# A retention stage with its output one chunk behind its state and scores, ahead of a mixture of experts

## The chip, the cores and the metric

The kernel runs on one core of one Trainium2 chip. The metric is the time of one execution on the device in microseconds (us). The time before is the median of three runs, 659.53 us (658.33 to 659.57).

## The reference

q, k and v are (2 batches, 8 heads, 576 positions, 64). Retention is attention with a decay in place of the softmax; a mixture of 4 experts and one more layer with a Mish-like activation follow.

```python
gamma = 1 - 2 ** (-5 - arange(H))                      # one decay per head
D = where(i >= j, gamma ** (i - j), 0)                 # i, j positions
x = matmul((q @ k.T) / 8 * D, v)                       # -> (1152 tokens, 512)
p = domain_probs / (domain_probs.sum(-1) + 1e-9)
x = sum(p[:, e] * (relu(x @ w1[e]) @ w2[e]) for e in range(4))   # 512 -> 1024 -> 512
h = x @ w_in                                           # 512 -> 2048
out = (h * tanh(softplus(h))) @ w_out                  # 2048 -> 512
```

## The kernel before

**The stages.** The program has two stages. The retention stage goes through 18 chunks of 64 tokens (9 for each batch). The matrix stage works through 144 tiles of 128 hidden features by 384 tokens, each with 12 matmuls into a hidden bank and then 12 that project it (`project`, `project_tokens`). Each product of two fp32 numbers is made of three matmuls of rounded parts (`three`, lines 314 to 316): hi by hi, hi by lo, lo by hi. For each weight tile ("half") ACT makes the part w_hi (`unit_hi`, L212) and POOL then w_lo (`unit_lo`, L218); for the tokens ACT makes x_hi (L442) and VectorE x_lo (L494).

**One chunk.** `qkv` has 8 slots. The first 64 partitions (KEYS) of a slot hold v and k by position; the other 64 (FEATS) hold k and q by feature. TensorE multiplies k and q for the scores (`scores_head`, L268), into one of two banks. POOL multiplies v by its decay (`v_decay`, L636), for which it needs the chunk and the constants. VectorE masks the scores and writes them over k in the slot (`masked`, L479), once the state's matmuls have read k. The state is the running sum of k times v, one matmul per head (`state_head`, L272), accumulated in bank 2 over a batch. ACT copies it into the next slot over k by feature (`state_copy`, L409), once the next chunk's scores have read that. So a slot then holds state over v and q over masked scores, and the output is one matmul per head with 128 rows (`output`, L308). VectorE scales it to `x_tmp` (`decayed`, L488), ACT and VectorE split it in x_hi and x_lo (`first_lo`). `row_decay` (L591) makes a table that the scaling uses, one row ahead.

**The order.** Each engine's queue is written out by hand and runs in order, with semaphores between them. TensorE's turn c (L386 to L391) is: scores of chunk c+1 with the state of chunk c, head by head in alternation (`scores_and_state`); output of chunk c. From turn 7 on, halves of hidden tiles of the matrix stage (`hidden_half`, 6 matmuls each) stand in it, after the scores (AFTER_SCORES) and after the output (AFTER_OUTPUT): two a turn in turns 7 to 11, one in turns 12 to 17. VectorE's turn c is masked(c), a row of row_decay, first_lo(c-1), the hidden tiles' work (`lo`, `moe_act`), decayed(c). ACT's turn c is state_copy(c), x_hi(c-1), in turn 2 a wait for the probabilities' write and a DMA, then the w_hi that SPLIT_IN gives this turn and the h_hi. POOL's turn c is v_decay(c+1) and then the w_lo of SPLIT_IN, weight tiles 0 to 7 in turns 6 to 12. The SP queue loads chunk 0, the constants (214 KB), chunks 1 to 6, weight tiles 0 and 1, and then chunks and weight tiles in turn; from chunk 8 on each chunk waits for the output of the chunk 8 before it.

**Its end.** After turn 17 TensorE does a whole hidden tile (`hidden_products(8)`), and the first `project` waits for a drain of VectorE (L604) behind decayed(17), first_lo(17) and moe_act(7).

Of the kernel before, what the change touches and what calls it, by code (L numbers as in the profile page):

```python
# [13 lines left out]
P = 128  # L14
# [28 lines left out]

ROW0 = PAIRS * CH
STEP0 = ROW0 + PER_BATCH * PAIRS
KEY0 = STEP0 + PER_BATCH * HEADS
CONSTS = KEY0 + CH

# [5 lines left out]
def states(c):  # L54
# [3 lines left out]

AFTER_SCORES = {7: (0, 0), 8: (1, 0), 9: (2, 0), 10: (3, 0), 11: (4, 0),
                12: (5, 0), 13: (5, 1), 14: (6, 0), 15: (6, 1), 16: (7, 0), 17: (7, 1)}
AFTER_OUTPUT = {7: (0, 1), 8: (1, 1), 9: (2, 1), 10: (3, 1), 11: (4, 1)}
HIDDEN_IN = {t: c for turns in (AFTER_SCORES, AFTER_OUTPUT) for c, (t, half) in turns.items() if half}

SPLIT_IN = {0: 6, 1: 6, 2: 7, 3: 8, 4: 9, 5: 10, 6: 11, 7: 12, 8: 16, 9: 17, 10: 18}

# [14 lines left out]
def build(nc, chunks_in, consts_in, probs_in, weights_in, probs_dram, out):  # L82
    with ExitStack() as ctx:
# [41 lines left out]

        row0 = consts[:, 0:ROW0].rearrange("p (h c) -> p h c", h=PAIRS)
        row_step = consts[:, ROW0:STEP0].rearrange("p (c h) -> p c h", h=PAIRS)
        key_decay = consts[:, STEP0:KEY0].rearrange("p (c h) -> p c h", h=HEADS)
        mask = consts[KEYS, KEY0:CONSTS]

        banks = [ctx.enter_context(nc.psum_tensor(f"bank{i}", [P, 512], F32)) for i in range(8)]
        ps_s = [banks[i][KEYS, :].rearrange("p (h c) -> p h c", h=HEADS) for i in range(2)]
        ps_state = banks[2][FEATS, :].rearrange("p (h c) -> p h c", h=HEADS)
        ps_o = banks[3][:, 0:PAIRS * CH].rearrange("p (h c) -> p h c", h=PAIRS)
# [4 lines left out]
        s_slot = [sem(f"s_slot{i}") for i in range(SLOTS)]  # L139
        s_const = sem("s_const")  # L140
        s_zt = sem("s_zt")
        s_vd = sem("s_vd")
# [81 lines left out]
        def _(sp):  # L224
# [10 lines left out]
            load_chunk(0)  # L235
            sp.dma_start(consts[:, :], consts_in).then_inc(s_const, 16)
            for c in range(1, 7):
                load_chunk(c)
            load_half(0)
            for u in range(1, UNITS):  # L240
                load_half(u)
                load_chunk(6 + u)
# [23 lines left out]
        def _(pe):  # L266
            def scores_head(c, h):
                return pe.matmul(ps_s[c % 2][:, h], by_feats(c, 0)[:, h], by_feats(c, 1)[:, h],  # L268
                                 start=True, stop=True)

            def state_head(c, h):
                return pe.matmul(ps_state[:, h], by_keys(c, 1)[:, h], by_keys(c, 0)[:, h],  # L272
                                 start=(c % PER_BATCH == 0 and h == 0), stop=True, skip_group_check=True)

            def scores_and_state(c):

                n = c + 1
                if n < CHUNKS:
                    pe.wait_ge(s_slot[n % SLOTS], landed(n))
                    if n >= 2:  # L280
                        pe.wait_ge(s_sm, n - 1)
                if has_state(c):
                    pe.wait_ge(s_vd, c + 1)
                    if c > 0:
                        pe.wait_ge(s_st, states(c - 1))
                for h in range(HEADS):
                    if n < CHUNKS:
                        mm = scores_head(n, h)
                        if h == HEADS - 1:
                            mm.then_inc(s_sc, 1)  # L290
                    if has_state(c):
                        mm = state_head(c, h)
                        if h == HEADS - 1:
                            mm.then_inc(s_kv, 1)

            def output(c):

                pe.wait_ge(s_vd, c + 1)
                pe.wait_ge(s_sm, c + 1)
                rows = KEYS  # L300
                if c % PER_BATCH > 0:
                    rows = slice(0, P)
                    pe.wait_ge(s_st, states(c - 1))
                if c > 0:
                    pe.wait_ge(s_xt, c)
                for hp in range(PAIRS):
                    for x in range(2):
                        mm = pe.matmul(ps_o[DH * x:DH * (x + 1), hp], qkv[rows, c % SLOTS, 0, 2 * hp + x],  # L308
                                       qkv[rows, c % SLOTS, 1, 2 * hp + x], start=True, stop=True)
                mm.then_inc(s_o, 1)  # L310
# [73 lines left out]
            mm.then_inc(s_sc, 1)  # L384
            for c in range(CHUNKS):
                scores_and_state(c)  # L386
                if c in AFTER_SCORES:
                    hidden_half(*AFTER_SCORES[c])
                output(c)
                if c in AFTER_OUTPUT:  # L390
                    hidden_half(*AFTER_OUTPUT[c])  # L391
# [10 lines left out]
        def _(act):  # L402
# [3 lines left out]
            def state_copy(c):  # L406
                act.wait_ge(s_sc, c + 2)
                act.wait_ge(s_kv, states(c))
                act.activation(by_feats(c + 1, 0), ps_state, ACT.Copy).then_inc(s_st, 1)  # L409

# [25 lines left out]

            for c in range(CHUNKS + 1):
                if c < CHUNKS and has_state(c):
                    state_copy(c)
                if c > 0:  # L440
                    act.wait_ge(s_xt, c)
# [31 lines left out]
        def _(dve):  # L473
            def masked(c):

                dve.wait_ge(s_sc, c + 1)
                if has_state(c):
                    dve.wait_ge(s_kv, states(c))
                dve.tensor_tensor(by_keys(c, 1), ps_s[c % 2], mask.unsqueeze(1).broadcast_to([CH, HEADS, CH]),  # L479
                                  ALU.mult).then_inc(s_sm, 1)  # L480
# [105 lines left out]

            for c in range(CHUNKS + 1):
                if c < CHUNKS:
                    masked(c)
                if c < PER_BATCH - 1:  # L590
                    dve.tensor_tensor(row_decay[:, c + 1], row0,  # L591
                                      row_step[:, c + 1].unsqueeze(2).broadcast_to([P, PAIRS, CH]), ALU.mult)\
                       .then_inc(s_rd, 1)
                if c > 0:
                    first_lo(c - 1)
                for t, turn in HIDDEN_IN.items():
                    if turn + 2 == c:
                        lo(t)
                for t, turn in HIDDEN_IN.items():
                    if turn + 1 == c:  # L600
                        moe_act(t)
                if c < CHUNKS:
                    decayed(c)
            dve.drain().then_inc(s_af, KT)  # L604
# [55 lines left out]
def tables():  # L660
# [3 lines left out]
    c = np.arange(PER_BATCH, dtype=np.float64)  # L664
    consts = np.zeros((P, CONSTS))
    rows = gamma[:, None] ** (i[None, :] - MID) / np.sqrt(DH)
    consts[:, 0:ROW0] = np.repeat(rows.reshape(PAIRS, 2, CH).transpose(1, 0, 2), DH, axis=0).reshape(P, ROW0)
    steps = gamma[:, None] ** (CH * c[None, :])
    steps = np.repeat(steps.reshape(PAIRS, 2, PER_BATCH).transpose(1, 2, 0), DH, axis=0)
    consts[:, ROW0:STEP0] = steps.reshape(P, STEP0 - ROW0)  # L670
    keys = gamma[None, None, :] ** (MID - CH * c[None, :, None] - i[:, None, None])
    consts[KEYS, STEP0:KEY0] = keys.reshape(CH, KEY0 - STEP0)
    consts[KEYS, KEY0:CONSTS] = i[:, None] <= i[None, :]
    return consts.astype(np.float32)
# [32 lines left out]
```

## Time and profile before

| | |
|---|---|
| median of three runs | 659.53 us (658.33 to 659.57) |
| profiled execution | 655.74 us, of it 653.9 us span |
| TensorE (PE) busy | 638.8 us, 98% |
| VectorE (DVE) busy | 357.3 us, 55% |
| ScalarE (ACT), GpSimd (POOL) | 219.7 us, 204.4 us |
| granted TensorE clock | 0.999 of full speed |
| retention stage | to about 65.4 us |

PE is TensorE's matmuls, PEld its weight loads, which overlap them. Times in the trace count from the start of the span. A matmul's end is modelled and matmuls overlap, so of a run of them the starts are what to read. A fp32 matmul leaves two records: 8 matmuls show as x16. In a row "[2.90 <-DMA x]" is idle time of the engine ahead of the instruction and what ended it.

### The profile page before, as it was taken

What the parts mean: (1) busy time and instruction counts of PE and PEld (TensorE: products, weight loads), DVE (VectorE), ACT (ScalarE), POOL (GpSimd) and SP (SyncE); (2) the same over time, 40 slices, a digit from 0 to 9 for tenths busy, and PEclk for the clock granted to TensorE, in tenths of its full rate; (3) what the DMA queues carried; (4) which work ended last, traced back from release to release, by engine and by line L of the source; (5) the groups of instructions that cost most, each with busy time, mean ns of one, the idle gap of its engine ahead of it and who ended that gap; (6) DMA issues with size and microseconds to landing.
All of it is one profiled execution on the core that took longest, in us unless ns stands there. A gap on an engine that the chain in (4) does not pass through costs nothing.

```text
span 653.9 us, 10358 instructions
## 1 busy us (share of the span) xinstructions
PE 638.8 (98%) x4153; PEld 609.8 (93%) x4153; DVE 357.3 (55%) x624; ACT 219.7 (34%) x431; POOL 204.4 (31%) x167
## 2 busy tenths in 40 slices
PE   6799999999999999999999999999999999999998
PEld 4688999999999999999999999999998999999986
DVE  4757333232423232424242324348999999999772
ACT  2445312222212212212212212336554655565540
POOL 5464402222212212211212211224443555553220
PEclk9999999999999999999999999999999999999999
DMA  8854311111111201111111110111110111001001
GB/s 335 337 187 143 97 33 49 49 34 49 49 33 33 65 33 48 50 33 34 48 49 49 50 32 25 57 33 34 48 49 17 49 48 34 2 1 48 1 33 65
DMA packets 19232, 40.25 MB, mean 62 GB/s; under 512 B 2672, under 2 KB 2928, under 8 KB 19184
## 3 DMA queue, kind: packets, MB, share of 16 engines
q1 hardware_dynamic: 18368, 39.35, 19.1%
q8 instruction: 33, 0.54, 0.3%
q10 hardware_dynamic: 816, 0.23, 0.2%
q14 instruction: 15, 0.12, 0.1%
HBM read 37.20 MB, written 2.38 MB: 61 GB/s over the span
## 4 chain that ended last, share of the span: by engine, by line
PE 85%; DVE 9%; DMA 2%; issue 2%; ACT 1%; POOL 0%; SPq 0%; ACTq 0%; DVEq 0%
PE bank L314 28%; PE bank L316 27%; PE bank L315 27%; DVE m_n L568 2%; PE bank L268 2%; DVE m_a L556 1%; DVE m_w L558 1%; DMA probs_by_expert<-p_norm 1%; PE bank L308 1%; DVE m_c L565 1%; DVE h_lo L500 1%; DMA qkv<-in_chunks 1%; DVE x_lo L547 1%; DVE acc_sb L542 0%; ACT qkv L409 0%
## 5 line engine op out<-in xcount | busy, mean ns | idle before, releaser
L218 POOL TENSOR_TENSOR w_lo<-w_raw,w_hi 128x512 fp32r<-128x512 f32 x96 | 129.5, 1350 | 305.1 <-ACT w_hi L212 305.1
L314 PE MATMUL bank<-x_hi,w_hi 128*128 128x384 f32 x576 | 194.7, 338 | 0.5 <-POOL w_lo L218 0.5
L316 PE MATMUL bank<-x_hi,w_lo 128*128 128x384 f32 x576 | 193.0, 335 | 0.0
L315 PE MATMUL bank<-x_lo,w_hi 128*128 128x384 f32 x576 | 192.7, 335 | 0.0
L416 ACT ACTIVATE h_hi<-h_act 128x384 fp32r<-128x384 f32 x144 | 75.6, 525 | 305.7 <-PE bank L316 266.6
L500 DVE TENSOR_TENSOR h_lo<-h_act,h_hi 128x384 fp32r<-128x384 f32 x144 | 83.4, 579 | 164.5 <-ACT h_hi L416 163.8
L314 PE MATMUL bank<-h_hi,w_hi 128*128 128x384 f32 x384 | 128.3, 334 | 0.0
L315 PE MATMUL bank<-h_lo,w_hi 128*128 128x384 f32 x384 | 128.3, 334 | 0.0
L316 PE MATMUL bank<-h_hi,w_lo 128*128 128x384 f32 x384 | 128.3, 334 | 0.0
L314 PEld LDWEIGHTS bank<-x_hi,w_hi 128*128 128x128 f32 x576 | 108.1, 188 | 3.4 <-issue 0.6
L315 PEld LDWEIGHTS bank<-x_lo,w_hi 128*128 128x128 f32 x576 | 108.1, 188 | 1.7
L316 PEld LDWEIGHTS bank<-x_hi,w_lo 128*128 128x128 f32 x576 | 108.1, 188 | 0.0
L513 DVE SCALAR_TENSOR_TENSOR h_act<-bank,pb 128x384 f32<-128x384 f32 x96 | 53.4, 557 | 78.2 <-PE bank L316 78.2
L642 POOL TENSOR_TENSOR m_t<-m_w,m_r 128x384 f32<-128x384 f32 x48 | 55.6, 1159 | 117.3 <-ACT m_r L435 117.3
L314 PEld LDWEIGHTS bank<-h_hi,w_hi 128*128 128x128 f32 x384 | 72.1, 188 | 0.2 <-issue 0.2
L315 PEld LDWEIGHTS bank<-h_lo,w_hi 128*128 128x128 f32 x384 | 72.1, 188 | 0.0
L316 PEld LDWEIGHTS bank<-h_hi,w_lo 128*128 128x128 f32 x384 | 72.1, 188 | 0.0
L212 ACT ACTIVATE w_hi<-w_raw 128x512 fp32r<-128x512 f32 x96 | 59.1, 618 | 17.8 <-PE bank L316 17.8
L314 PE MATMUL bank<-w_hi,h_hi 128*128 128x512 f32 x144 | 56.2, 390 | 1.3 <-DVE acc_sb L540 1.1
L316 PE MATMUL bank<-w_hi,h_lo 128*128 128x512 f32 x144 | 56.8, 395 | 0.0
L315 PE MATMUL bank<-w_lo,h_hi 128*128 128x512 f32 x144 | 56.7, 394 | 0.0
L558 DVE SCALAR_TENSOR_TENSOR m_w<-m_u,m_a 128x384 f32<-128x384 f32 x48 | 42.4, 882 | 1.7
(42 smaller groups left out, 492.8 us busy)
## 6 DMA issues: line engine op xcount, KB each, us to landing
w_raw<-in_weights SPq DMA_DIRECT2D x96, 256.0 KB, 2.7
qkv<-in_chunks SPq DMA_DIRECT2D x18, 512.0 KB, 6.6
pb<-probs_by_expert SPq DMA_DIRECT2D x3, 576.0 KB, 6.0
out<-acc_sb SPq DMA_DIRECT2D x2, 768.0 KB, 4.5
out<-acc_sb SPq DMA_DIRECT2D x3, 256.0 KB, 2.1
pb<-probs_by_expert SPq DMA_DIRECT2D x1, 384.0 KB, 5.3
consts<-in_consts SPq DMA_DIRECT2D x1, 214.0 KB, 3.8
pb<-probs_by_expert ACTq DMA_DIRECT2D x1, 192.0 KB, 7.1
```

What stands on the lines that cost most here:

```text
L212: act.activation(w_hi[:, part, u], w_raw[:, half % RAW], ACT.Copy).then_inc(s_wh, 1)
L218: pool.tensor_tensor(w_lo[:, part, u], w_raw[:, half % RAW], w_hi[:, part, u].bitcast(F32), ALU.subtract).then_inc(s_wl, 1)
L268: return pe.matmul(ps_s[c % 2][:, h], by_feats(c, 0)[:, h], by_feats(c, 1)[:, h], start=True, stop=True)
L314: pe.matmul(out, w[0], x[0], start=first, stop=False)
L315: pe.matmul(out, w[0], x[1], start=False, stop=False)
L316: return pe.matmul(out, w[1], x[0], start=False, stop=last)
L416: act.activation(h_hi[:, n % UNITS, :], h_act[:, n % 2, :], ACT.Copy).then_inc(s_hh, 1)
L500: dve.tensor_tensor(h_lo[:, n % UNITS, :], h_act[:, n % 2, :], h_hi[:, n % UNITS, :].bitcast(F32), ALU.subtract).then_inc(s_hl, 1)
L513: dve.scalar_tensor_tensor(h_act[:, n % 2, :], ps_h[n % HR], 0.0, pb[:, e, cols(c)], ALU.max, ALU.mult).then_inc(s_hf, 1)
L558: dve.scalar_tensor_tensor(m_w[:, n % 2, :], m_u[:, n % 2, :], MISH_CAP, m_a[:, :], ALU.min, ALU.mult).then_inc(s_w, 1)
L568: dve.scalar_tensor_tensor(m_n[:, :], m_c[:, :], 2.0, m_t[:, n % 2, :], ALU.subtract, ALU.mult).then_inc(s_mn, 1)
L642: pool.tensor_tensor(m_t[:, n % 2, :], m_w[:, n % 2, :], m_r[:, n % 2, :], ALU.mult).then_inc(s_t, 1)
```

## The change

TensorE's turn c issues the output of chunk c-1 rather than c, so there are 19 turns. The hidden halves, ACT's and VectorE's turns follow by one. Scores have three banks (0 to 2) rather than two. The state lies in banks 0 and 1 (four heads each, on the partitions that the scores don't use) rather than bank 2, ACT copies it in two instructions, and TensorE waits for the first ahead of head 0 and for the second ahead of head 4. VectorE does decayed(c-1) right behind masked(c), and row_decay and first_lo after it. The constants load in two DMAs: key decay and mask (64 partitions, 35 KB) ahead of chunk 1, the rest behind it. Weight tile 0 is loaded ahead of chunk 6, and split in turn 5. Of the diff, the function that lays out the constants' table on the host is left out.

```diff
--- before.py
+++ after.py
@@ -41,10 +41,11 @@
 MISH_CAP = float(np.exp(20.0))
 
 
-ROW0 = PAIRS * CH
-STEP0 = ROW0 + PER_BATCH * PAIRS
-KEY0 = STEP0 + PER_BATCH * HEADS
-CONSTS = KEY0 + CH
+
+MASK0 = PER_BATCH * HEADS
+ROW0 = MASK0 + CH
+STEP0 = ROW0 + PAIRS * CH
+CONSTS = STEP0 + PER_BATCH * PAIRS
 
 
 def has_state(c):
@@ -57,13 +58,18 @@
 
 
 
-
-AFTER_SCORES = {7: (0, 0), 8: (1, 0), 9: (2, 0), 10: (3, 0), 11: (4, 0),
-                12: (5, 0), 13: (5, 1), 14: (6, 0), 15: (6, 1), 16: (7, 0), 17: (7, 1)}
-AFTER_OUTPUT = {7: (0, 1), 8: (1, 1), 9: (2, 1), 10: (3, 1), 11: (4, 1)}
+TURNS = CHUNKS + 1
+SCORES = 3
+HS = HEADS // 2
+
+
+
+AFTER_SCORES = {8: (0, 1), 9: (1, 1), 10: (2, 1), 11: (3, 1), 12: (4, 1), 13: (5, 0), 14: (5, 1),
+                15: (6, 0), 16: (6, 1), 17: (7, 0), 18: (7, 1)}
+AFTER_OUTPUT = {7: (0, 0), 8: (1, 0), 9: (2, 0), 10: (3, 0), 11: (4, 0)}
 HIDDEN_IN = {t: c for turns in (AFTER_SCORES, AFTER_OUTPUT) for c, (t, half) in turns.items() if half}
 
-SPLIT_IN = {0: 6, 1: 6, 2: 7, 3: 8, 4: 9, 5: 10, 6: 11, 7: 12, 8: 16, 9: 17, 10: 18}
+SPLIT_IN = {0: 5, 1: 6, 2: 7, 3: 8, 4: 9, 5: 10, 6: 11, 7: 12, 8: 16, 9: 17, 10: 18}
 
 
 def split_steps():
@@ -123,14 +129,14 @@
         m_c = sb("m_c", [P, TC])
         m_n = sb("m_n", [P, TC])
 
-        row0 = consts[:, 0:ROW0].rearrange("p (h c) -> p h c", h=PAIRS)
-        row_step = consts[:, ROW0:STEP0].rearrange("p (c h) -> p c h", h=PAIRS)
-        key_decay = consts[:, STEP0:KEY0].rearrange("p (c h) -> p c h", h=HEADS)
-        mask = consts[KEYS, KEY0:CONSTS]
+        key_decay = consts[:, 0:MASK0].rearrange("p (c h) -> p c h", h=HEADS)
+        mask = consts[KEYS, MASK0:ROW0]
+        row0 = consts[:, ROW0:STEP0].rearrange("p (h c) -> p h c", h=PAIRS)
+        row_step = consts[:, STEP0:CONSTS].rearrange("p (c h) -> p c h", h=PAIRS)
 
         banks = [ctx.enter_context(nc.psum_tensor(f"bank{i}", [P, 512], F32)) for i in range(8)]
-        ps_s = [banks[i][KEYS, :].rearrange("p (h c) -> p h c", h=HEADS) for i in range(2)]
-        ps_state = banks[2][FEATS, :].rearrange("p (h c) -> p h c", h=HEADS)
+        ps_s = [banks[i][KEYS, :].rearrange("p (h c) -> p h c", h=HEADS) for i in range(SCORES)]
+        ps_state = [banks[i][FEATS, 0:HS * DH].rearrange("p (h c) -> p h c", h=HS) for i in range(2)]
         ps_o = banks[3][:, 0:PAIRS * CH].rearrange("p (h c) -> p h c", h=PAIRS)
         ps_acc = [banks[d][:, 0:TC] for d in range(KT)]
         ps_out = [banks[tt][:, :] for tt in range(TT)]
@@ -138,6 +144,7 @@
 
         s_slot = [sem(f"s_slot{i}") for i in range(SLOTS)]
         s_const = sem("s_const")
+        s_rows = sem("s_rows")
         s_zt = sem("s_zt")
         s_vd = sem("s_vd")
         s_sc = sem("s_sc")
@@ -233,11 +240,12 @@
                 sp.dma_start(w_raw[:, half % RAW], weights_in[half]).then_inc(s_raw[half % RAW], 16)
 
             load_chunk(0)
-            sp.dma_start(consts[:, :], consts_in).then_inc(s_const, 16)
-            for c in range(1, 7):
+            sp.dma_start(consts[KEYS, 0:ROW0], consts_in[KEYS, 0:ROW0]).then_inc(s_const, 16)
+            load_chunk(1)
+            sp.dma_start(consts[:, ROW0:], consts_in[:, ROW0:]).then_inc(s_rows, 16)
+            for c in range(2, 6):
                 load_chunk(c)
-            load_half(0)
-            for u in range(1, UNITS):
+            for u in range(UNITS):
                 load_half(u)
                 load_chunk(6 + u)
             for c in range(6 + UNITS, CHUNKS):
@@ -265,25 +273,25 @@
         @block.tensor
         def _(pe):
             def scores_head(c, h):
-                return pe.matmul(ps_s[c % 2][:, h], by_feats(c, 0)[:, h], by_feats(c, 1)[:, h],
+                return pe.matmul(ps_s[c % SCORES][:, h], by_feats(c, 0)[:, h], by_feats(c, 1)[:, h],
                                  start=True, stop=True)
 
             def state_head(c, h):
-                return pe.matmul(ps_state[:, h], by_keys(c, 1)[:, h], by_keys(c, 0)[:, h],
-                                 start=(c % PER_BATCH == 0 and h == 0), stop=True, skip_group_check=True)
+                return pe.matmul(ps_state[h // HS][:, h % HS], by_keys(c, 1)[:, h], by_keys(c, 0)[:, h],
+                                 start=(c % PER_BATCH == 0 and h % HS == 0), stop=True, skip_group_check=True)
 
             def scores_and_state(c):
 
                 n = c + 1
                 if n < CHUNKS:
                     pe.wait_ge(s_slot[n % SLOTS], landed(n))
-                    if n >= 2:
-                        pe.wait_ge(s_sm, n - 1)
+                    if n >= SCORES:
+                        pe.wait_ge(s_sm, n - SCORES + 1)
                 if has_state(c):
                     pe.wait_ge(s_vd, c + 1)
-                    if c > 0:
-                        pe.wait_ge(s_st, states(c - 1))
                 for h in range(HEADS):
+                    if has_state(c) and c > 0 and h % HS == 0:
+                        pe.wait_ge(s_st, 2 * states(c - 1) - 1 + h // HS)
                     if n < CHUNKS:
                         mm = scores_head(n, h)
                         if h == HEADS - 1:
@@ -300,7 +308,7 @@
                 rows = KEYS
                 if c % PER_BATCH > 0:
                     rows = slice(0, P)
-                    pe.wait_ge(s_st, states(c - 1))
+                    pe.wait_ge(s_st, 2 * states(c - 1))
                 if c > 0:
                     pe.wait_ge(s_xt, c)
                 for hp in range(PAIRS):
@@ -382,11 +390,13 @@
             for h in range(HEADS):
                 mm = scores_head(0, h)
             mm.then_inc(s_sc, 1)
-            for c in range(CHUNKS):
-                scores_and_state(c)
+            for c in range(TURNS):
+                if c < CHUNKS:
+                    scores_and_state(c)
                 if c in AFTER_SCORES:
                     hidden_half(*AFTER_SCORES[c])
-                output(c)
+                if c > 0:
+                    output(c - 1)
                 if c in AFTER_OUTPUT:
                     hidden_half(*AFTER_OUTPUT[c])
             for n in range(TILES):
@@ -406,7 +416,9 @@
             def state_copy(c):
                 act.wait_ge(s_sc, c + 2)
                 act.wait_ge(s_kv, states(c))
-                act.activation(by_feats(c + 1, 0), ps_state, ACT.Copy).then_inc(s_st, 1)
+                for i in range(2):
+                    at = by_feats(c + 1, 0)[:, HS * i:HS * (i + 1)]
+                    act.activation(at, ps_state[i], ACT.Copy).then_inc(s_st, 1)
 
             def hi(n):
 
@@ -434,10 +446,10 @@
                 act.wait_ge(s_ln, n - MOE_TILES + 1)
                 act.activation(m_r[:, n % 2, :], m_r[:, n % 2, :], ACT.Exp, scale=-1.0).then_inc(s_r, 1)
 
-            for c in range(CHUNKS + 1):
+            for c in range(TURNS + 1):
                 if c < CHUNKS and has_state(c):
                     state_copy(c)
-                if c > 0:
+                if 0 < c <= CHUNKS:
                     act.wait_ge(s_xt, c)
                     act.activation(x_hi[:, :, CH * (c - 1):CH * c], x_tmp[:, (c - 1) % 2], ACT.Copy).then_inc(s_xh, 1)
                 if c == 0:
@@ -476,7 +488,7 @@
                 dve.wait_ge(s_sc, c + 1)
                 if has_state(c):
                     dve.wait_ge(s_kv, states(c))
-                dve.tensor_tensor(by_keys(c, 1), ps_s[c % 2], mask.unsqueeze(1).broadcast_to([CH, HEADS, CH]),
+                dve.tensor_tensor(by_keys(c, 1), ps_s[c % SCORES], mask.unsqueeze(1).broadcast_to([CH, HEADS, CH]),
                                   ALU.mult).then_inc(s_sm, 1)
 
             def decayed(c):
@@ -584,23 +596,25 @@
                .then_inc(s_pc, 1)
             dve.wait_ge(s_const, 16)
 
-            for c in range(CHUNKS + 1):
+            for c in range(TURNS + 1):
                 if c < CHUNKS:
                     masked(c)
+                if c == 0:
+                    dve.wait_ge(s_rows, 16)
+                if 0 < c <= CHUNKS:
+                    decayed(c - 1)
                 if c < PER_BATCH - 1:
                     dve.tensor_tensor(row_decay[:, c + 1], row0,
                                       row_step[:, c + 1].unsqueeze(2).broadcast_to([P, PAIRS, CH]), ALU.mult)\
                        .then_inc(s_rd, 1)
-                if c > 0:
-                    first_lo(c - 1)
                 for t, turn in HIDDEN_IN.items():
                     if turn + 2 == c:
                         lo(t)
                 for t, turn in HIDDEN_IN.items():
                     if turn + 1 == c:
                         moe_act(t)
-                if c < CHUNKS:
-                    decayed(c)
+                if 0 < c <= CHUNKS:
+                    first_lo(c - 1)
             dve.drain().then_inc(s_af, KT)
 
             for n in range(TILES):
...
```

## Rows read from the trace of the kernel before

**Rows 1.** The page, part 1: busy time, share of the span and instructions by engine.

```profile
PE 638.8 (98%) x4153; PEld 609.8 (93%) x4153; DVE 357.3 (55%) x624; ACT 219.7 (34%) x431; POOL 204.4 (31%) x167
```

**Rows 2.** Busy time by stretch: length, PE, PEld, DVE, ACT, POOL, clock, DMA share, GB/s.

```profile
8.40:10.95 2.55, 1.61 (x48) 1.51 (x48) 1.70 (x3) 0.57 (x1) 2.06 (x3) 1.00 1.01 413
...
16.34:19.57 3.23, 1.83 (x48) 1.62 (x48) 1.77 (x4) 1.01 (x2) 1.31 (x1) 1.00 1.03 410
...
32.34:36.52 4.18, 4.18 (x61) 3.54 (x61) 1.91 (x5) 1.46 (x3) 2.93 (x3) 1.00 0.40 124
...
65.44:67.73 2.29, 2.29 (x13) 2.11 (x14) 1.48 (x4) 1.21 (x3) 1.95 (x2) 1.00 0.51 119
67.73:653.90 586.17, 581.65 (x3204) 562.12 (x3204) 314.86 (x543) 191.89 (x378) 169.43 (x134) 1.00 0.14 40
```

**Rows 3.** TensorE's waits, 66 to 654 us: total us, times, longest.

```profile
PE bank L314 <- DVE acc_sb L540: 1.1, 1, 1.1
PE bank L314 <- DVE acc_sb L542: 0.2, 1, 0.2
```

**Rows 4.** TensorE's waits, 27.7 to 66 us.

```profile
PE bank L308 <- DVE qkv L479: 0.7, 1, 0.7
PE bank L314 <- POOL w_lo L218: 0.5, 1, 0.5
```

**Rows 5.** The chain of waits in order of time: start, us, what.

```profile
18.33 0.24 PE bank L268
...
23.06 0.69 PE bank L308 x16
...
28.11 0.41 PE bank L314
...
29.41 0.62 PE bank L308 x16
...
31.27 1.07 PE bank L268 x16
```

**Rows 6.** ACT in order of time: start, us, line, operation, tiles [idle before].

```profile
8.40 0.38 ACTq L445 DMA_DIRECT2D probs_by_expert<-p_norm  x1
...
17.59 0.59 ACT L409 ACTIVATE qkv<-bank 64x512 f32<-64x512 f32 x1 [2.90 <-DMA probs_by_expert<-p_norm]
...
37.27 0.42 ACT L442 ACTIVATE x_hi<-x_tmp 128x256 fp32r<-128x256 f32 x1
37.60 0.62 ACT L212 ACTIVATE w_hi<-w_raw 128x512 fp32r<-128x512 f32 x1
...
56.28 0.42 ACT L442 ACTIVATE x_hi<-x_tmp 128x256 fp32r<-128x256 f32 x1 [0.58 <-DVE x_tmp L488]
```

**Rows 7.** DMA issues, first 75 us: KB each, median us to landing.

```profile
probs_by_expert<-p_norm ACTq DMA_DIRECT2D x1, 18.0 KB, 8.7
```

**Rows 8.** VectorE in order of time.

```profile
23.86 0.42 DVE L488 TENSOR_TENSOR x_tmp<-bank,row_decay 128x256 f32<-128x256 f32 x1
...
29.60 2.49 DVE L494 TENSOR_TENSOR x_lo<-x_tmp,x_hi 128x256 fp32r<-128x256 f32 x1
...
53.30 1.30 DVE L494 TENSOR_TENSOR x_lo<-x_tmp,x_hi 128x256 fp32r<-128x256 f32 x1 [0.45 <-ACT x_hi L442]
...
55.83 0.41 DVE L488 TENSOR_TENSOR x_tmp<-bank,row_decay 128x256 f32<-128x256 f32 x1
```

**Rows 9.** POOL in order of time.

```profile
26.69 2.70 POOL L218 TENSOR_TENSOR w_lo<-w_raw,w_hi 128x512 fp32r<-128x512 f32 x2 [8.42 <-ACT w_hi L212]
29.36 1.22 POOL L636 TENSOR_TENSOR qkv<-qkv,consts 64x512 f32<-64x512 f32 x1
...
38.29 1.49 POOL L218 TENSOR_TENSOR w_lo<-w_raw,w_hi 128x512 fp32r<-128x512 f32 x1 [2.54 <-ACT w_hi L212]
39.73 1.04 POOL L636 TENSOR_TENSOR qkv<-qkv,consts 64x512 f32<-64x512 f32 x1
...
52.27 4.54 POOL L636 TENSOR_TENSOR qkv<-qkv,consts 64x512 f32<-64x512 f32 x4
```

More of the change, by code:

```diff
@@ L665, in tables @@
     consts = np.zeros((P, CONSTS))
+    keys = gamma[None, None, :] ** (MID - CH * c[None, :, None] - i[:, None, None])
+    consts[KEYS, 0:MASK0] = keys.reshape(CH, MASK0)
+    consts[KEYS, MASK0:ROW0] = i[:, None] <= i[None, :]
     rows = gamma[:, None] ** (i[None, :] - MID) / np.sqrt(DH)
-    consts[:, 0:ROW0] = np.repeat(rows.reshape(PAIRS, 2, CH).transpose(1, 0, 2), DH, axis=0).reshape(P, ROW0)
+    consts[:, ROW0:STEP0] = np.repeat(rows.reshape(PAIRS, 2, CH).transpose(1, 0, 2), DH, axis=0).reshape(P, -1)
     steps = gamma[:, None] ** (CH * c[None, :])
     steps = np.repeat(steps.reshape(PAIRS, 2, PER_BATCH).transpose(1, 2, 0), DH, axis=0)
[L670 to L673, printed above, removed]
+    consts[:, STEP0:CONSTS] = steps.reshape(P, CONSTS - STEP0)
     return consts.astype(np.float32)
```

## The prediction, made before the result

> **What bounds the kernel now.** I read the page first: TensorE is busy for 98% of the span, the others for 55% or less [rows 1]. Then the busy time by stretch: from 67.73 us to the end the matrix stage runs 586.17 us [rows 2], and there TensorE waits only 1.1 and 0.2 us [rows 3]. The change touches nothing of that stage but the moment at which it starts. So I read the retention stage by turns. A turn is one pass of TensorE's loop; I write S(c) for the scores of chunk c+1 and state of chunk c, O(c) for the output, H for a hidden half (6 matmuls). The early turns take 2.55 to 2.8 us, with TensorE busy for 1.61 to 1.9; the one that ends at 19.57 takes 3.23; from 32.34 on, four turns in a row take 4.18 to 4.20 and TensorE is busy throughout [rows 2]. After 27.7 us it waits twice, 0.5 us for POOL's w_lo and 0.7 us for the mask of chunk 14 [rows 4]. All that a better order can win lies before 28.11 us, where the first H starts [rows 5], plus this 0.7.
>
> **The durations.** S takes 1.07 us to issue: at 31.27 us the 16 records are scores alone, and the turns with state too are no longer, so the two ride side by side. O takes 0.69 alone (23.06) and 0.61 where matmuls follow (29.41 to 30.02), an H 1.25 (from there to 31.27) [rows 5]. 1.25+1.07+1.25+0.61 = 4.18, the turn above.
>
> **The early turns: what goes.** Before, O(c) stands between S(c) and S(c+1) and waits for the mask of its own chunk, the 0.9 us in which TensorE idles. Afterwards O(c-1) finds its mask done a turn earlier. The new loop is S(c), copy of the state, S(c+1): 1.07 to issue, 0.09 for the last to end, 0.12 to ACT (my estimate from the way back), the first copy piece, 0.14 back (17.59+0.59 to 18.33) [rows 5, 6]. A copy of 64x256 isn't in the trace. Its bounds are 0.42 (128x256, x_hi) and 0.59 (64x512, the whole copy) [rows 6]; the width is that of the first, so I take 0.41. The turn becomes 1.83 us, and O(c-1), 0.61, lies in the wait of 0.76. The second piece is issued 0.33 behind and is ready before head 4, which comes 0.53 into S. It costs nothing there; if pieces took 0.59, a turn would be 0.18 longer.
>
> **What is late next: the small write.** ACT issues the write of the normalised probabilities at 8.40 and at turn 2 waits until it has landed, 8.7 us later. Only then come another DMA and, at 17.59, the copy of state 3, after 2.90 us of waiting [rows 6, 7]; that is why this turn is the one of 3.23 us [rows 2]. The change leaves this wait where it is. The smaller constants ahead of chunk 1 save 179 KB, at 413 GB/s [rows 2] 0.45 us, so S(0) ends about that much sooner; the write stands behind two copy pieces and goes out 0 to 0.35 us sooner, say 0.25. The SP queue has as much in flight as before, so I leave 8.7 us. State copy 3 starts at 17.34 rather than 17.59. The turns 0 to 3, which the change makes some 0.9 us shorter each, end in this wait, and their gain is lost but for 0.25.
>
> From there: S(4) 17.90 to 18.97, S(5) 19.73 to 20.80, O(4) to 21.41, S(6) 21.56 to 22.63, O(5) to 23.24. Without more, S(7) would start at 23.3 against about 26.5 before.
>
> **What stops it: the decay of the values, on POOL behind a weight part.** POOL runs the decay of chunk c+1 and then the w_lo of the turn, in order. In turn 5 that is w_lo(0), and the decay of chunk 7, which S(7) waits for, stands behind it. w_lo(0) waits for ACT's w_hi(0), which stands behind x_hi(4), which waits for the scaling of O(4). Before, x_hi of a turn followed the state copy at once, since its output was of the turn before; now it comes after O(c-1) of the same turn. The chain has its pieces in the trace: from the end of O's issue 0.19 to x_tmp (23.06+0.61 to 23.86), 0.45 from there to x_hi (55.83 to 56.28), 3.50 from x_hi's start to the decay's end (37.27, 37.60, 38.29, 39.73+1.04), 0.13 back to TensorE (26.69, two parts of 1.29 on end, to the H at 28.11 that wants the first is the nearest row: 0.13): 4.27 us [rows 5, 6, 8, 9]. In turn 5 VectorE is late as well: mask 5 at 21.10, x_tmp(4) 21.71, x_hi(4) 22.16, w_hi(0) 22.49, w_lo(0) 23.18, the decay 24.45 to 25.67 (1.22, the length of the one behind a w_lo at 29.36). S(7) runs from 25.80, O(6) ends at 27.48, and the first H starts then, against 28.11: **0.63 us won**. What is left of the list (16 H, 9 S, 11 O) is the same from there on in both.
>
> **The same chain again at turn 12.** Turns with two H hide it: from the end of O(k) to S(k+3) lie 5.4 us, more than 4.27. From O(10) to S(13) it is 4.18: 0.09 lost. In turn 12 the last w_lo, part 7, waits for O(11) by this chain, and the decay of chunk 14 stands behind it. Up to S(14) TensorE has S(13), one H and O(12): 1.07+1.25+0.61 = 2.93. **It waits 4.27-2.93 = 1.34 us.** Before, the decay of chunk 14 started at 52.27 and ended near 53.4 [rows 9], and S(14) came only after that (TensorE's busy stretch has no wait there, [rows 4]). Bounds by the lengths of the w_lo (1.27 to 1.49) and the decay (1.03 to 1.22) [rows 9]: 1.1 to 1.5; if the phase of POOL falls otherwise, 0.
>
> **The wait for mask 14 goes**: O(14) comes a turn after its mask, **0.7 us won** [rows 4].
>
> **The end of the stage.** The first projection starts 2.29 us after O(17) (65.44 to 67.73) [rows 2], behind x_lo(17), moe_act and a drain. Now lo(6) stands between x_tmp(17) and x_lo(17), while POOL runs w_lo parts 9 and 10. VectorE operations with two SBUF inputs are held up while POOL works: x_lo took 2.49 at 29.60 and 1.30 at 53.30 instead of 0.42 [rows 8, 9]. I take **0.3 lost**, between 0 and 1.4.
>
> The remaining edits I cost at nothing. The third score buffer loosens a wait that never shows [rows 4]. TensorE's wait at head 4 has the 0.3 us just worked out. The slots come free one turn later in turns that are shorter: chunk 8 waits for O(0), which ends near 10.2, and is needed after 23. Half 0 ahead of chunk 6 delays that by 0.64 us (256 KB), to about 14.1 by my count from 413 GB/s, needed at 21.5. Moving row_decay and x_lo behind x_tmp costs nothing new; VectorE is busy for 1.77 us in the turn of 3.23 [rows 2], and a turn has 1.83.
>
> **The sum**: -0.63 - 0.7 + 1.34 + 0.09 + 0.3 = +0.4 us on 655.74 of the profiled execution (its span 653.9), so 656.1. The median of the runs shown is 659.53, 3.8 above the profiled one; I add the difference to it: **659.9 us, no change that a measurement can tell** (about 0.2%, 1.3 us).
>
> **A rule weighed.** State and scores use the two row halves of the array side by side and write bank 2 and bank 0 or 1, in 1.07 us for both or for one [rows 5]; now they share bank 0 or 1 in part of the turns. The outputs share bank 3 between column halves, but each takes all rows (in the first chunk of a batch the same half), so no row shows this case. The Trainium skill ("TensorEngine Tiling (Array Packing)", Gotcha 1: PSUM Pressure) says that different row tiles cannot access the same PSUM bank simultaneously. No run here shows it yet; it is a rival below.
>
> **The rivals.**
> A, faster: the chain through POOL doesn't bite, or half as much, since w_hi gets out sooner than I think. Without it S(7) starts 2.5 us sooner and S(14) 1.4 sooner: 0.4-3.9 = -3.5, **656.0 us**; half of it gives 658.0. For it: POOL is idle 8.42 us ahead of w_lo(0) [rows 9], so there is room. Against it: the program order on ACT and POOL. 18%.
> B, slower: shared banks run one after the other. A turn shares where (c+1) mod 3 is 0 or 1 and has state: four heads at 1.07/8 = 0.134, 0.54 us. It decides after the small write: once in the early turns (S(5)) and five times later: 3.2 us. With the 0.4: +3.6, **663.1 us**. 9%.
> C, slower: VectorE is starved. x_lo(5) comes due at 24.7, amid w_lo(0), the decay of 7, w_lo(1) and the decay of 8, back to back until 28.1. If it loses the port at two changes, it ends at 28.4 and the first H, which wants it, starts 0.9 late; with the 1.4 at the end instead of 0.3 that is +2.4, **661.9 us**. For it: 2.49 us at 29.60. Against: at 53.30 it lost only one. 15%.
> That the change doesn't bring its early gain is in the forecast itself: 58%, with a range of its own from 658.3 to 661.5.
>
> **How the numbers follow.** Faster: A's 18% and 8% of the forecast's spread (the small write landing a microsecond sooner, or POOL in another phase at turn 12): 26%. Slower: B 9%, C 12%, 7% of the forecast: 28%. Same: 46%. The range takes in C, the forecast, the dearer copy piece (+0.4) and half of A: 656.4 to 662.6; outside are B and the better half of A.
>
> **What would show it.** Right: ACT's wait for the small write grows from 2.9 to 5 us or more and copy 3 starts near 17.3; turns after it take 1.8 us; the decay of 7 starts past 24 us behind w_lo(0) with TensorE idle over 2 us ahead of S(7); a gap of about 1.3 us ahead of S(14); no wait of O for a mask. Wrong: S longer than 1.07 us where banks are shared (B), the first H later than 28 us waiting for x_lo (C), the first H before 26 us (A).

## The result

| | before | changed |
|---|---|---|
| median | 656.08 us (20 executions, 655.64 to 660.92) | 660.03 us (20, 657.73 to 663.65) |
| profiled execution | 655.74 us, span 653.9 | 659.61 us, span 657.8 |
| mean granted clock in it | 0.999 | 0.992 |

The ratio is 1.0048 (95% interval 1.0032 to 1.0063): slower by about half a per cent, some 3 us. I had forecast no change: +0.4 us. The 659.9 on record was near the measured time only because the first three executions of the kernel before (median 659.53) lay 3.5 us above its median over 20. Two profiled executions compare one with the other: +3.9 us, where the sum had +0.4.

The page of the changed kernel, its engine row and two rows of part 2 (slices of a fortieth of the span): the second digit of PEclk has fallen to 7. In the clock row of the kernel before every slice was 9.

```profile
PE 642.5 (98%) x4153; PEld 612.8 (93%) x4153; DVE 356.3 (54%) x624; ACT 220.5 (34%) x447; POOL 202.8 (31%) x167
PE   7799999999999999999999999999999999999998
PEclk9799999999999999999999999999999999999999
```

Busy time by stretch (columns as in [rows 2]: PE, PEld, DVE, ACT, POOL, clock, DMA share, GB/s). The third number from the end, the clock, tells the story. It is 1.00 up to 14.10. TensorE is then idle until 18.40, the clock falls within that stretch, and what follows runs at 0.50 to 0.52, the 1.2 GHz level. TensorE is idle again for most of 25.2 to 28.0; S(7) right behind it still runs at 1.00, and the O and the first H after that at 0.55. The matrix stage is what it was.

```profile
12.00:14.10 2.10, 1.85 (x54) 1.62 (x48) 1.99 (x5) 0.69 (x2) 1.21 (x2) 1.00 1.06 383
14.10:18.40 4.30, 0.12 (x5) 0.00 (x0) 1.45 (x4) 0.43 (x2) 1.03 (x1) 0.70 1.05 409
...
18.40:20.50 2.10, 2.01 (x34) 1.92 (x36) 0.43 (x1) 0.64 (x2) 0.00 (x0) 0.50 1.02 408
20.50:22.70 2.20, 2.20 (x40) 2.08 (x42) 1.60 (x4) 1.07 (x3) 0.00 (x0) 0.52 0.95 344
...
25.20:28.00 2.80, 0.33 (x12) 0.20 (x9) 2.80 (x4) 1.62 (x5) 2.69 (x3) 1.00 0.86 301
28.00:29.16 1.16, 1.14 (x34) 1.09 (x36) 1.16 (x1) 0.00 (x0) 1.16 (x2) 1.00 0.82 316
29.16:32.19 3.03, 3.03 (x24) 2.47 (x24) 2.56 (x6) 1.59 (x4) 1.64 (x2) 0.55 0.47 144
...
71.00:657.00 586.00, 582.09 (x3206) 562.33 (x3204) 314.91 (x544) 192.12 (x378) 169.67 (x134) 1.00 0.14 40
```

TensorE's waits in the first 70 us (total, times, longest), where [rows 4] stood. The mask's wait is gone. Two new ones stand there: for the state copy (4.3) and for the decay of the values (2.5, and 1.1 ahead of S(14)).

```profile
PE bank L276 <- ACT qkv L421: 4.4, 2, 4.3
PE bank L276 <- POOL qkv L650: 3.6, 2, 2.5
```

ACT in order of time answers to [rows 6]: the write is issued at 8.12 and ACT waits 4.13 us for it where it had waited 2.90. Then POOL: w_lo(0) waits for ACT, and the decay of chunk 7 stands behind it; at 53.78 the same with w_lo(7) and the decay of chunk 14.

```profile
8.12 0.38 ACTq L457 DMA_DIRECT2D probs_by_expert<-p_norm  x1
...
17.97 0.65 ACT L421 ACTIVATE qkv<-bank 64x256 f32<-64x256 f32 x2 [4.13 <-DMA probs_by_expert<-p_norm]
```

```profile
25.32 1.27 POOL L225 TENSOR_TENSOR w_lo<-w_raw,w_hi 128x512 fp32r<-128x512 f32 x1 [8.56 <-ACT w_hi L219]
26.54 1.22 POOL L650 TENSOR_TENSOR qkv<-qkv,consts 64x512 f32<-64x512 f32 x1
...
53.78 1.36 POOL L225 TENSOR_TENSOR w_lo<-w_raw,w_hi 128x512 fp32r<-128x512 f32 x1 [1.84 <-ACT w_hi L219]
55.09 4.53 POOL L650 TENSOR_TENSOR qkv<-qkv,consts 64x512 f32<-64x512 f32 x4
```

The chain in order of time, in place of [rows 5]. The copy of state 3 comes at 17.97 and x_tmp(4) at 23.86. S(7) starts at 28.02 and O(6) takes 0.80. In the first H the matmuls come 0.32 apart instead of 0.17, S(8) takes 1.39, and the H at 33.58 is at full speed again. S(10) takes 1.08 (40.87 to 41.95) and so does S(11) (45.06 to 46.14). At 56.38 comes S(14).

```profile
17.97 0.39 ACT qkv L421
...
23.86 0.42 DVE x_tmp L500
...
28.02 0.24 PE bank L276
29.16 0.80 PE bank L316 x16
29.97 0.62 PE bank L322
30.59 0.32 PE bank L323
...
32.19 1.39 PE bank L276 x16
33.58 0.37 PE bank L322
...
40.87 0.20 PE bank L276
...
41.95 0.38 PE bank L322
...
45.06 0.20 PE bank L276
...
46.14 0.38 PE bank L322
...
51.57 0.64 PE bank L316 x16
...
56.38 0.24 PE bank L276
...
68.38 0.64 PE bank L316 x16
...
71.43 0.41 PE bank L322
```

The ledger between the two traces: the first H 1.86 us later (28.11 to 29.97); that H and S(8) at the lower clock, 3.61 us (29.97 to 33.58) where 1.25+1.07 = 2.32 would do, 1.29; the mask's wait -0.7; the wait ahead of S(14) +1.1 to 1.3. That is 3.55 to 3.75, and the last output starts 3.63 later (64.75 to 68.38).

### The profile page after: what moved, and what is told of

It reads as the page before. It is cut to its first block, busy times and chain, and to the rows that moved or that the text cites. A ratio compares the mean times of both kernels' runs of the same rounds, so it can differ in the third digit from the quotient of the medians.

```text
span 657.8 us, 10374 instructions
## 1 busy us (share of the span) xinstructions
PE 642.5 (98%) x4153; PEld 612.8 (93%) x4153; DVE 356.3 (54%) x624; ACT 220.5 (34%) x447; POOL 202.8 (31%) x167
## 4 chain that ended last, share of the span: by engine, by line
PE 86%; DVE 9%; DMA 2%; issue 1%; ACT 1%; POOL 1%; DVEq 0%; SPq 0%; ACTq 0%
PE bank L322 28%; PE bank L324 27%; PE bank L323 27%; DVE m_n L580 2%; PE bank L276 2%; DVE m_a L568 1%; DMA probs_by_expert<-p_norm 1%; DVE m_w L570 1%; PE bank L316 1%; DVE m_c L577 1%; DVE h_lo L512 1%; DMA qkv<-in_chunks 1%; DVE x_lo L559 1%; DVE acc_sb L554 0%; PE bank L280 0%
```

## The experiments

Each is compared with executions of the kernel before on the same chip, whose median was 655.97 to 656.33. "Full clock" is a mean granted clock of 0.999 or 1.

| kernel | median us | ratio to before (95%) |
|---|---|---|
| changed | 660.03 | 1.0048 (1.0032 to 1.0063) |
| old banks, one-piece copy | 659.33 | 1.0059 (1.0031 to 1.0087) |
| one gap filled | 657.66 | 1.0006 (0.9982 to 1.0029) |
| both gaps filled | 658.53 | 1.0023 (1.0005 to 1.0042) |
| w_lo behind the decay | 659.29 | 1.0017 (0.9995 to 1.0038) |
| small write waited for late | 656.09 | 0.9973 (0.9956 to 0.9991) |
| both moves | 654.26 | 0.9945 (0.9923 to 0.9966) |
| + lighter loads | 653.29 | 0.9957 (0.9935 to 0.9979) |
| + later splits | 652.83; again 652.50 | 0.9941 (0.9919 to 0.9963); 0.9926 (0.9906 to 0.9947) |
| before, late wait | 655.87 | 0.9986 (0.9968 to 1.0003) |
| before, with moves and lighter loads | 656.10 | 0.9995 (0.9975 to 1.0015) |

**One gap filled.**

```diff
+FILL = {4: 18}
...
+                for _ in range(FILL.get(c, 0)):
+                    pe.matmul(banks[7][:, :], zeros[:, 0:P], zeros[:, :], start=True, stop=True)
                 if c < CHUNKS:
                     scores_and_state(c)
```

> The changed kernel with 18 matmuls of zeros (128x512 bf16, into an unused bank) put on TensorE ahead of turn 4, where it stands idle for 4.3 us for the copy of state 3. Nothing else waits for them. Theory (clock): the idle time itself made the granted clock fall to 0.5 from 18.4 to 22.7 us, and the fill keeps it up: S(4) takes 1.07 us again rather than 2.0, the first H starts near 28.1 rather than 29.97, and if the clock then also holds through the first H, the span falls by 1.9 to 3.2 us against the changed kernel. Rival (shared banks or the copy in two pieces make S slow): S(4) stays at 2 us and the time stays within 0.3 us of the changed kernel, or grows.

Its stretches, to set beside those above. With TensorE kept busy through the same wait, the clock of the next 4.3 us is 1.00:

```profile
14.10:18.40 4.30, 4.17 (x25) 1.72 (x20) 1.69 (x4) 0.00 (x0) 1.04 (x1) 1.00 1.05 396
18.40:22.70 4.30, 3.58 (x98) 3.26 (x99) 2.61 (x6) 2.71 (x8) 0.00 (x0) 1.00 1.04 394
25.20:28.00 2.80, 2.06 (x45) 1.89 (x42) 1.80 (x4) 1.58 (x4) 1.69 (x3) 0.74 0.83 280
28.00:31.00 3.00, 3.00 (x37) 2.60 (x34) 1.59 (x4) 1.26 (x4) 1.91 (x2) 0.67 0.38 120
```

S(4), by TensorE's groups from 18.3 to 20.6 us, first filled, then as changed. The idle time falls from 4.3 to 0.8 and the mean matmul from 0.31 to 0.22 us:

```profile
L277 PE MATMUL bank<-qkv 64*64 64x64 f32 x16 | 1.1, 219 | 0.8 <-ACT qkv L424 0.8
```

```profile
L276 PE MATMUL bank<-qkv 64*64 64x64 f32 x16 | 1.9, 313 | 4.3 <-ACT qkv L421 4.3
```

The chain at the two places named above, the copy of state 3 and x_tmp(4):

```profile
18.57 0.39 ACT qkv L424
...
22.83 0.42 DVE x_tmp L503
```

So the idle stretch lowers the clock, and the clock made S slow. S(4) says nothing of shared banks, since its scores go to bank 2 and the state to banks 0 and 1. S(5) does share bank 0, and here it takes 1.08 (20.87 to 21.95), as S(4) does (19.10 to 20.18). The median fell by 2.4. The first H came no sooner in this trace (29.82, forecast 28.1): TensorE paused 1.4 us in the midst of S(6) (23.64 to 25.00) for nothing the profile names, and the clock fell once, later.

**Both gaps filled**: FILL = {4: 18, 7: 11}.

> The changed kernel with fills in both gaps: 18 zero matmuls ahead of turn 4 as in the kernel with one fill, and 11 ahead of turn 7, where TensorE waits 1.2 to 2.5 us for the decay of chunk 7. Theory (clock): no stretch at the lower clock is left, the first H runs at 1.25 to 1.3 us; 1 to 1.7 us below the kernel with one fill (657.7), so 656 to 656.7, no better than the kernel before, since the waits themselves stay. Rival (the clock falls in any case once in the run): within 0.5 us of the kernel with one fill.

No lower stretch is left in the profiled execution, and 7 of 11 ran at full clock. Yet the median is 658.53: above the one fill, against the forecast of 1 to 1.7 less. The second fill takes 2.48 us and ends after the decay that S(7) wants (the decay ends at 26.04, S(7) starts at 27.77), so it pays with its own length. Its executions at full clock take 657.65 to 658.74, and before had 655.44 to 656.4 in most of its own. These 2 us are the waits and the fill that runs over, without the clock; this kernel doesn't tell the two apart. What the clock costs is better read from the one fill, which gave back 2.4 us of the median and still had one lower stretch in its trace.

**Old banks, one-piece copy.**

```diff
-SCORES = 3
+SCORES = 2
...
-        ps_state = [banks[i][FEATS, 0:HS * DH].rearrange("p (h c) -> p h c", h=HS) for i in range(2)]
+        ps_state = banks[2][FEATS, :].rearrange("p (h c) -> p h c", h=HEADS)
...
-                for i in range(2):
-                    at = by_feats(c + 1, 0)[:, HS * i:HS * (i + 1)]
-                    act.activation(at, ps_state[i], ACT.Copy).then_inc(s_st, 1)
+                act.activation(by_feats(c + 1, 0), ps_state, ACT.Copy).then_inc(s_st, 1)
```

> The changed kernel with the banks of the kernel before: two score buffers, the state in bank 2 alone, copied in one piece of 64x512; the lag, the loads and all else as changed. Theory (these edits carry nothing, since the small write and POOL's order set the early turns): within 1 us of the changed kernel (660.0), the turn 0.2 us longer. Rival B of the prediction (shared banks cost): 2 us or more below the changed kernel, with S shorter in it.

659.33 against 660.03, with overlapping intervals (its ten executions spread from 657.55 to 666.16): banks and pieces carry nothing that can be measured here, in either direction. Rival B wanted 2 us or more below the changed kernel, and is out.

**The small write waited for late.**

```diff
-                if c == 2:
+                if c == 6:
                     act.wait_ge(s_ps, 16)
```

> The changed kernel with ACT's wait for the small write (and the DMA behind it) in turn 6 rather than turn 2. Theory (the write holds up the copy of state 3, and idle time lowers the clock): turns 3 to 6 follow each other at 1.8 to 2 us, S(7) still waits for the decay of chunk 7 behind w_lo(0) but at about 22 us rather than 28, the first H starts near 24; 4.5 to 6 us less than the changed kernel, so 1.5 to 3 us less than the kernel before. Rival (the loads are as late: chunks and weight tile 0 come at 410 GB/s and hold the turns): the first H not before 27, under 3 us gained.

The first H starts at 24.62, 5.35 us sooner, and the median is 3.9 below the changed kernel, less than the 4.5 to 6 of the forecast. The wait ahead of S(14) stays, S(7) doesn't wait for its decay, and a new stop shows in the midst of O(5) (chain in order of time):

```profile
19.48 0.49 PE bank L316 x11
19.98 2.56 issue
22.54 0.39 PE bank L316 x5
```

**w_lo behind the decay**: on POOL each w_lo comes one turn later, behind that turn's decay.

```diff
-                    if turn == c:
+                    if turn + 1 == c or (turn == c == 18):
                         unit_lo(pool, half)
```

> The changed kernel with POOL's w_lo of each turn moved behind the next turn's decay, so that no decay of values stands behind a w_lo that waits for ACT. ACT's wait for the small write stays. Theory (POOL's order causes the waits of TensorE ahead of S(7), 2.5 us, and S(14), 1.1 to 1.4 us): both go, the first H starts near 27 and its clock stays at 1.0; 4 to 5.4 us less than the changed kernel. Rival (chunk 7's decay would be late anyway, or the first H then waits for w_lo(0) instead): S(7) early but the first H still past 28.5, under 2.5 us gained.

The waits for the decay are gone, but the first H (28.46) now waits 1.8 us for x_lo(5). Neither theory nor rival named that: the rival had it wait for w_lo(0). It is rival C of the prediction. TensorE's waits, and the chain at that place:

```profile
PE bank L276 <- ACT qkv L421: 5.1, 3, 4.2
PE bank L322 <- DVE x_lo L506: 1.8, 1, 1.8
```

```profile
25.23 0.77 DVE row_decay L607
26.00 2.41 DVE x_lo L506
```

The executions fall in two groups: four at 655.65 to 656.43 (clock 0.994 to 0.997) and eight at 658.77 to 660.25 (0.990 to 0.992). One kernel, two times, told apart by the clock.

**Both moves.**

> The changed kernel with both: ACT's wait for the small write in turn 6, and each w_lo behind the next turn's decay. Theory: the early turns run at 1.8 to 2 us without a wait over 1 us, the first H starts between 20 and 22 us at full clock, no wait ahead of S(14): 8 to 9.5 us less than the changed kernel, 5 to 6 less than before. Rival (transfers bind next: by the bytes ahead of them chunk 8 lands near 18 and each later chunk with its weight tile 1.9 us after): first H at 23 or later, 6 to 7 us less than the changed kernel.

654.26: 5.8 below the changed kernel and 2 below before, less than either theory. The pause in O(5) is here as well, 2.39 us from 19.94, and after it TensorE ran at 0.50:

```profile
PE bank L316 <- issue: 2.4, 1, 2.4
```

```profile
20.00:22.00 2.00, 0.00 (x0) 0.00 (x0) 0.46 (x1) 0.61 (x2) 1.99 (x2) 0.94 1.00 393
22.00:24.00 2.00, 1.67 (x27) 1.55 (x29) 0.83 (x3) 0.52 (x2) 0.27 (x1) 0.50 1.04 405
```

**Lighter loads**: weight tiles 3 to 7 behind chunk 13.

```diff
             for u in range(UNITS):
+                if u < 3:
+                    load_half(u)
+                load_chunk(6 + u)
+            for u in range(3, UNITS):
                 load_half(u)
-                load_chunk(6 + u)
```

> The kernel with both moves (ACT's wait in turn 6, each w_lo behind the next decay), and weight tiles 3 to 7 loaded behind chunk 13 instead of between the chunks, so that the load queues run dry near 19 us. In the kernel with both moves TensorE stood still for 2.39 us in the midst of O(5), at 19.94, with nothing in the profile that it waited for, until 1.0 us after a 16 KB packet of the instruction queue (20.22 to 21.32). Theory (that packet is the next block of TensorE's code, late behind the saturated loads): the pause shrinks below 1 us, the clock keeps its full level, the first H starts near 20 to 21 rather than 24, and the time falls by 2 to 4.5 us, to 650 to 652. Rival (the pause belongs to the place in the code whatever the loads do): it stays at 2.4 us and the time within 1 us of that kernel's 654.3.

The long pause is gone (O at 22.16 takes 1.04 instead of 0.69, 0.35 over). That the lighter loads took it away isn't shown: the DMA engines are still busy for 0.98 of the time from 20 to 21 us, and TensorE reaches this place (about 22.65) a microsecond after the end of the instruction packet (20.57 to 21.62), where with both moves it came at 19.94, ahead of it (20.22 to 21.32). Executions at full clock take 651.38 to 653.68. But here x_lo(5) took 2.48 us, the first H waited 1.8 for it, and four of twelve executions took 655.9 to 657.2. Median 653.29.

**Later splits**: SPLIT_IN for tiles 1 to 7 one turn later, for a hole in POOL's work.

> The kernel with both moves and the lighter loads, and weight tiles 1 to 7 split one turn later (SPLIT_IN 7 to 13 instead of 6 to 12), tile 0 as before. In the one without this POOL ran w_lo(0), a decay, w_lo(1) and a decay back to back from 22.97 to 27.8 us, x_lo(5) took 2.48 us in it, and TensorE waited 1.8 us for it and then ran 6.8 us at the lower clock. Theory (rival C of the prediction, VectorE starved by POOL): POOL has a hole behind the decay of chunk 8, x_lo(5) ends at least 1.2 us sooner, TensorE's wait for it falls below 0.8 us, the executions at the lower clock become rare, and the median falls by 0.5 to 2 us to 651.5 to 652.8. Rival (the clock falls from the light load of the early turns themselves, or the later w_lo makes the next H wait): the same spread from 651.4 to 657 and the median within 0.5 us of 653.3, or above.

x_lo took 1.19 and the H's wait fell to 0.7; all seven executions lie between 652.35 and 653.19. The median gained 0.5, the least of what was forecast and too little to be told from nothing. The pause is back at 1.32 us, after the same eleventh record of an output as in the two kernels with 2.4 and 2.6. In this kernel and without the later splits the loads are equally light, but here TensorE reaches the place at 21.30, before the packet's end (21.46), and there well after it.

```profile
20.77 0.53 PE bank L319 x11
21.30 1.32 issue
...
24.21 1.19 DVE x_lo L509
...
25.45 0.45 PE bank L325
```

**Before, late wait.**

> The kernel before with ACT's wait for the small write in turn 6 rather than turn 2, no other change. Theory: its copy of state 3 comes at 16.4 rather than 17.6, so turn 3 is 0.5 us shorter (2.7 instead of 3.23) and each later one starts so much sooner; 0.5 us less, within noise (same). Rival (the wait costs the kernel before a fall of the clock in some executions): over 1 us less, with its spread to 659.7 gone.

655.87 against 656.28, interval across 1: the same. Its executions at the lower clock remain. Its five fastest (654.62 to 654.89, at full clock) lie below every one of the kernel before (655.44 at the least), by about what the half microsecond of the forecast would give.

**Before, with moves and lighter loads; the best once more.** The last two ran in the same rounds.

> The kernel before (output of its own chunk, two score buffers, one state copy) with the moves that made the changed kernel faster: ACT's wait for the small write in turn 6, each w_lo behind the next turn's decay, weight tiles 3 to 7 loaded behind chunk 13. Theory (the lag is worth something once nothing else holds the early turns): the early turns stay at 2.7 us, since each output waits for its own mask, the first H starts near 27.2 rather than 25.4, and the median is 654.8 to 655.9, 2 to 3 us above the lagged kernel with all moves (652.8). Rival (the moves alone bring it, the lag nothing): 652.5 to 653.5.

> The lagged kernel with all moves and the later splits once more, on the same chip and in the same rounds as the one without the lag. It should come at 652.8 again, 652.3 to 653.3, under the kernel before by 0.5 to 0.6%.

656.10 without the lag (forecast 654.8 to 655.9) and 652.50 with it; the slowest execution with it (653.17) is below the fastest without (654.53). Without it outputs still wait for their masks, and its first H starts at 26.88; with it at 24.52.

```profile
PE bank L311 <- DVE qkv L482: 3.6, 4, 1.0
```

So the change is worth about 3.6 us once the waits behind it are gone. The two kernels differ in all of the change (lag, banks, pieces, the constants' loads, weight tile 0) and in the later splits as well; without these it had 653.29, on another chip, which leaves 2.8 us. Banks and pieces carried nothing above; that the rest of it is the lag is argued from the masks' waits (3.6 us in all, 0 with the lag), not shown apart. The moves without the change leave the median where it was, though the five fastest executions (654.53 to 654.74) lie below every one of the kernel before (655.30 at the least).

## Why the prediction was right and wrong

**The small write: right in kind, and the failed step.** I had the copy of state 3 at 17.34; it came at 17.97, since the write took 9.4 us rather than 8.7. ACT's wait grew to 4.13, not to the 5 or more that I had set as the sign. The step that failed is the sentence after: "the turns 0 to 3 ... end in this wait, and their gain is lost but for 0.25". I priced idle time ahead of a fixed date as worth nothing. It cost: S(4), O(3) and S(5) at the lower clock put x_tmp(4) at 23.86 (forecast 21.71). Of those 2.15 us 0.63 are the write's and the rest the clock's. The filled kernel shows it: with the same wait, no idle time and the clock at 1.00, x_tmp(4) comes 4.26 us behind the copy of state 3 (18.57 to 22.83; 4.37 was forecast), and in the changed kernel 5.89. The Trainium skill ("TensorE: Matmul & The Clock Gate", What's actually happening) says the array's clock is halved when TensorE has been idle and comes back after activity; this trace agrees, with 1.00 ahead of the idle 4.3 us and 0.50 behind it. The rule would have given the right sign, and I weighed another.

**POOL's order: right.** The decay of 7 stood behind w_lo(0) and TensorE waited 2.49 us for it (2.5 forecast), all 2.1 to 2.2 us later than written. The wait ahead of S(14) was listed as 1.1 (forecast 1.34, from 1.1 to 1.5). Taking w_lo out of the way removed both.

**The mask's wait: right**, 0.7 gone. **The end of the stage**: 0.07 (2.98 to 3.05 from the last O to the first projection), not 0.3.

**The turn of 1.83: right where nothing else held it.** In the changed kernel the copies of states 1 and 2 lie 1.77 apart (9.85 to 11.62). At the lower clock those of states 3, 4 and 5 lie 2.60 and 2.67 apart (17.97, 20.57, 23.24), and those of 5 and 6 2.02, where the copy (25.26) stood on ACT behind w_hi(0) (24.62 to 25.23). A copy piece took 0.38, below both bounds that I had set (0.42 and 0.59).

**The rule on shared banks**: S(11), whose scores share bank 0 with the state, takes 1.08, as S(10) does, whose scores lie in bank 2 (both above). The sentence of the Trainium skill that the prediction cites would have the two take turns; this trace doesn't show it, and the trace decides. Rival B had no ground in time.

**Rival C** did not come in the changed kernel: x_lo(5) lost the port at two changes and took 2.48 us at 26.79, but S(7) was so late that the H didn't wait. It came in two kernels where S(7) was early (w_lo behind the decay, lighter loads), with a wait of 1.8 us in each, and of 0.7 and 1.0 in the two runs with later splits.

Sizes: +0.4 forecast; +1.29 for the H and S(8) at the lower clock and +2.49 for a first H at 29.97 instead of 27.48, less 0.3 to 0.6 for the three terms that came out smaller, give the +3.9 of the profiled pair within a few tenths.

## What to carry over

When a change makes an engine reach a fixed wait sooner, the idle time in front of the wait grows, and on TensorE idle time has a price of its own behind the wait: look for the clock there, fill it or move the wait. Ask of each queue what stands behind an instruction that now waits longer: here a short decay behind a weight split. A reordering that looks worthless may be worth its full gain once the next two waits are gone; with them gone, the kernels without and with this one take 656.1 and 652.5.

## What the runs showed of the hardware

- One kernel in two groups of times by the granted clock: 655.65 to 656.43 and 658.77 to 660.25. Idle time of 2.4 to 2.6 us ahead of the same instruction was followed by 0.50 in one trace (both moves) and by 1.00 in another (late wait), so such a gap doesn't lower the clock each time.
- TensorE stops at one place of its program for 1.0 to 2.6 us in six kernels. In four (late wait, both moves, both runs with later splits) it is behind the eleventh record of O(5); with the 18 matmuls of the fill ahead of it, it is 16 records sooner, in the midst of S(6) (one fill, both fills). Each time a 16 KB packet of the instruction queue ended 1.0 to 1.25 us before TensorE went on (21.32 and 22.33; 21.29 and 22.54; 21.46 and 22.62; 20.36 and 21.41; 23.78 and 25.00; 23.09 and 24.23). So the stop is the longer, the sooner TensorE comes to the place; in the changed kernel it came there over a microsecond after the packet (23.89) and didn't stop. The packet before shows the same: it ends at 15.25 with the later splits, and TensorE stops from 15.24 to 16.34; with the late wait it ends at 14.08, and TensorE stops from 14.63 to 15.22. The Trainium skill ("Runtime: NRT & Kernel Launch", Instruction fetch mechanics) says that code comes in 16 KiB blocks by a queue of its own and that this is mostly hidden; here it was not, with the DMA engines busy for 0.97 or more of the time while the packet was under way. Whether idle queues would hide it no run shows. That it is TensorE's code is argued from these times, not shown apart.
- The kernel before has executions of 659.6 us at a clock of 1.000; what holds them up stays open.
